# Three loads per pair of heads: one transfer of 128 rows each in place of two of 48, and the last pair taken second

## What is computed

```
f = 1 / (1 + exp(-f_logit))                      # batch 4, heads 8, seq 768, head_dim 48
for t in range(S):
    state = f[:, :, t, :, None] * state + einsum('bhd,bhe->bhde', k[:, :, t], v[:, :, t])
    y[:, :, t] = einsum('bhd,bhde->bhe', q[:, :, t], state)
x = y, heads side by side                        # (4, 768, 384)
x = first mixing network(x)                      # theta, cos/sin, token mixing, channel mixing
out = second mixing network(x)                   # w_in, normalise, w_spatial, gate, w_out
```

## Time and profile before

| | us |
|---|---|
| Median of 3 runs | 608.71 (608.22 to 608.74) |
| Profiled execution | 608.3 |
| Its span in the trace | 606.4 |
| Attention, until the mixing network runs alone | 0 to about 118 |
| Mixing networks | about 118 to 606.4 |

### The profile page before, as it was taken

How to read it: one execution, slowest core, us unless ns; L and a number is a source line. 1 busy time by engine, 2 the same in 40 slices (tenths; PEclk the granted TensorE clock), 3 DMA queues, 4 the chain that set the end, 5 groups by cost and what they waited for, 6 DMA issues and landing times.

```text
span 606.4 us, 11881 instructions
## 1 busy us (share of the span) xinstructions
PE 576.7 (95%) x4226; PEld 554.7 (91%) x4226; DVE 365.8 (60%) x614; ACT 289.9 (48%) x509; POOL 35.9 (6%) x66
## 2 busy tenths in 40 slices
PE   0898999999999999999999999999999999999997
PEld 0888888799988999999999999999999999989997
DVE  7899999677685456544855576557055704570240
ACT  5798999656453425333544345225221623253112
POOL 3233333100000000000000000000000000000000
PEclk9898999999999999999999999999999999999999
DMA  7889899486010221122013741200130011001102
GB/s 190 209 236 244 248 246 288 126 276 232 2 40 28 79 91 39 38 66 91 1 44 116 284 146 38 79 1 0 53 105 1 0 39 39 0 2 40 39 1 80
DMA packets 31113, 58.74 MB, mean 97 GB/s; under 512 B 3680, under 2 KB 23136, under 8 KB 30688
## 3 DMA queue, kind: packets, MB, share of 16 engines
q1 hardware_dynamic: 31072, 58.21, 31.5%
HBM read 44.04 MB, written 14.16 MB: 96 GB/s over the span
## 4 chain that ended last, share of the span: by engine, by line
PE 63%; DVE 5%; issue 3%; ACT 1%; DVEq 0%; ACTq 0%
PE gate_ps L1074 16%; PE ringc L1074 11%; PE small_ps L1074 10%; PE theta_bank L1074 9%; PE mix_ps L1537 5%; PE mix_ps L1542 5%; PE mix_ps L1538 5%; PE mix_ps L1074 1%; DVE stats L2069 1%; DVE w_lo L79 1%; PE small_ps L1501 1%; DVE z_lo L79 0%; DVE ang L1651 0%; DVE ang L1648 0%; DVE u L1693 0%
## 5 line engine op out<-in xcount | busy, mean ns | idle before, releaser
L1537 PE MATMUL mix_ps<-w_hi,z_hi 128*128 128x384 f32 x288 | 98.8, 343 | 0.7 <-DVE u L1693 0.7
L1538 PE MATMUL mix_ps<-w_lo,z_hi 128*128 128x384 f32 x288 | 96.7, 336 | 0.0
L1542 PE MATMUL mix_ps<-w_hi,z_lo 128*128 128x384 f32 x288 | 73.5, 337 | 0.0
L1074 PE MATMUL gate_ps<-w_hi 128*128 128x384 f32 x192 | 64.2, 334 | 0.0
L1074 PE MATMUL gate_ps<-w_hi,w_lo 128*128 128x384 f32 x192 | 64.2, 334 | 0.0
L1074 PE MATMUL gate_ps<-w_lo,w_hi 128*128 128x384 f32 x192 | 64.1, 334 | 0.0
L74 ACT ACTIVATE g_hi<-gate 128x384 fp32r<-128x384 f32 x32 | 16.9, 527 | 81.6 <-DVE gate L2119 81.6
L2115 DVE TENSOR_TENSOR gate<-gate_ps,b_all 128x384 f32<-128x384 f32 x32 | 17.8, 557 | 62.5 <-PE gate_ps L1074 62.5
L1537 PEld LDWEIGHTS mix_ps<-w_hi,z_hi 128*128 128x128 f32 x288 | 54.1, 188 | 1.2 <-DVE u L1693 1.1
L1538 PEld LDWEIGHTS mix_ps<-w_lo,z_hi 128*128 128x128 f32 x288 | 54.2, 188 | 0.0
L1542 PEld LDWEIGHTS mix_ps<-w_hi,z_lo 128*128 128x128 f32 x288 | 51.9, 188 | 0.2 <-DVE z_lo L79 0.2
(11 more groups left out here) (161 smaller groups left out, 1411.7 us busy)
## 6 DMA issues: line engine op xcount, KB each, us to landing
f_raw<-in_fT_dram SPq DMA_DIRECT2D x32, 144.0 KB, 3.6
k_raw<-in_kT_dram SPq DMA_DIRECT2D x32, 144.0 KB, 3.2
q_raw<-in_qT_dram SPq DMA_DIRECT2D x32, 144.0 KB, 3.7
v_raw<-in_vC_dram SPq DMA_DIRECT2D x16, 288.0 KB, 4.1
xT<-y_sb SPq DMA_DIRECT2D x32, 144.0 KB, 3.5
xt<-xT SPq DMA_DIRECT2D x8, 576.0 KB, 4.1
w_raw<-in_wB_dram SPq DMA_DIRECT2D x6, 768.0 KB, 6.1
u<-xT SPq DMA_DIRECT2D x8, 576.0 KB, 5.1
```

The costliest lines, as they stand in the source:

```text
L1074: done = pe.matmul(out, a, b, start=(first and n == 0), stop=(last and n == len(terms) - 1))
L1537: pe.matmul(out, z, w_hi[:, weights_of[r]], start=(s == 0 and r == 0), stop=False)
L1538: pe.matmul(out, z, w_lo[:, weights_of[r]], start=False, stop=False)
L1542: last = pe.matmul(out, part(z_lo[i], r * DMODEL + d * 128, 128), w_hi[:, weights_of[r]], start=False, stop=(s == ST - 1 and r == 1))
```

## The change

`f_raw`, `k_raw` and `q_raw` get 128 partitions (`LOADED`). One transfer fills all of them. Its source is a pattern written by hand over the DRAM tensor: 2 (a step of 48 rows), then 64 rows, then 768 values, so head 0 and the first 16 rows of head 1 go to partitions 0 to 63, and head 1 and the first 16 rows of the next pair to partitions 64 to 127. The destination is 128 partitions of 768 values. For the last pair these 16 rows would lie behind the end of the tensor, so it is loaded by two plain transfers, of 64 and of 48 rows. It is taken as step 1; step 0 stays pair 0, and steps 2 to 15 take pairs 1 to 14 (`taken`). Values and stores use the same order of pairs, their transfers are otherwise as before. The clearing of `f_raw`, `k_raw` and `q_raw` and the waits for it go. The load semaphores count 16 per load instead of 32, and one transfer more for buffer 1 (`rows_count`). The engines still work on partitions 0 to 111.

```diff
+LOADED = 2 * HEAD_AT[1]
-        f_raw = main.take("f_raw", [ROWS, SEQ], 2)
+        f_raw = main.take("f_raw", [LOADED, SEQ], 2)
...
-        f_in = [Count(nc, sems, f"f_in{i}", 32) for i in range(2)]
+        f_in = [Count(nc, sems, f"f_in{i}", 16) for i in range(2)]
...
+        def rows_count(c, p, i):
+
+            return half_count(c[i], p, 2) + 16 * i
...
-            def rows(raw, src, name, sem, p, b):
+            def taken(p):
+
                 if p.reg is None and p.const < 2:
-                    sp.wait_ge(cleared[name], b + 1)
-                for hd in range(2):
-                    sp.dma_start(raw[b % 2][HEAD_AT[hd]:HEAD_AT[hd] + HDIM, :],
-                                 src[p.times(1), hd * HDIM:(hd + 1) * HDIM, :]).then_inc(sem[b % 2].h, 16)
+                    return (0, PAIRS - 1)[p.const]
+                return p.times(1, -1)
+
+            def rows(raw, src, sem, p, b):
+                if p.reg is None and p.const == 1:
+
+                    for at, n in ((0, HEAD_AT[1]), (HEAD_AT[1], HDIM)):
+                        sp.dma_start(raw[b % 2][at:at + n, :], src[taken(p), at * HDIM // HEAD_AT[1]:at * HDIM // HEAD_AT[1] + n, :])\
+                          .then_inc(sem[b % 2].h, 16)
+                    return
+                heads_and_next = bass.AP(src.tensor, 0, [[PAIR * SEQ, PAIRS - 1], [HDIM * SEQ, 2], [SEQ, HEAD_AT[1]], [1, SEQ]])
+                sp.dma_start(raw[b % 2][:, :], heads_and_next[taken(p), :, :, :]).then_inc(sem[b % 2].h, 16)
...
-                             vC[p.times(1), :, :, :].rearrange("h p x -> p h x")).then_inc(v_in[b].h, 16)
+                             vC[taken(p), :, :, :].rearrange("h p x -> p h x")).then_inc(v_in[b].h, 16)
...
-            for i in range(2):
-                pool.memset(f_raw[i][:, :], 10.0).then_inc(cleared["f"], 1)
...
-            for i in range(2):
-                dve.memset(k_raw[i][:, :], 0.0).then_inc(cleared["k"], 1)
-                dve.memset(q_raw[i][:, :], 0.0).then_inc(cleared["q"], 1)
...
-                dve.wait_ge(q_in[i].h, half_count(q_in[i], p, 2))
-                if first(p):
-                    dve.wait_ge(cleared["q"], 2)
+                dve.wait_ge(q_in[i].h, rows_count(q_in, p, i))
```

More of the change, by code:

```diff
@@ L136, in ps @@
             return [ctx.enter_context(nc.psum_tensor(f"{name}{i}", [128, 512], F32)) for i in range(n)]
-        f_raw = main.take("f_raw", [ROWS, SEQ], 2)
+        f_raw = main.take("f_raw", [LOADED, SEQ], 2)
         cap = main.take("cap", [ROWS, SEQ], 2)
-        q_raw = main.take("q_raw", [ROWS, SEQ], 2)
-        k_raw = main.take("k_raw", [ROWS, SEQ], 2)
+        q_raw = main.take("q_raw", [LOADED, SEQ], 2)
+        k_raw = main.take("k_raw", [LOADED, SEQ], 2)
         csum = main.take("csum", [ROWS, SEQ], 2)
@@ L160, in attention @@
         cnt = lambda name, per, ahead=AHEAD: Count(nc, sems, name, per, ahead)
-        f_in = [Count(nc, sems, f"f_in{i}", 32) for i in range(2)]
-        q_in = [Count(nc, sems, f"q_in{i}", 32) for i in range(2)]
-        k_in = [Count(nc, sems, f"k_in{i}", 32) for i in range(2)]
+        f_in = [Count(nc, sems, f"f_in{i}", 16) for i in range(2)]
+        q_in = [Count(nc, sems, f"q_in{i}", 16) for i in range(2)]
+        k_in = [Count(nc, sems, f"k_in{i}", 16) for i in range(2)]
         v_in = [Count(nc, sems, f"v_in{i}", 16) for i in range(4)]
@@ L190, in attention @@
         y_sbd = cnt("y_sbd", 2)
-        cleared = {name: sems.enter_context(nc.semaphore(f"{name}_cleared")) for name in "fqk"}
         rest_cleared = sems.enter_context(nc.semaphore("rest_cleared"))
@@ L233, in _ @@
             m["open"]()
-            def rows(raw, src, name, sem, p, b):
+            def taken(p):
                 if p.reg is None and p.const < 2:
-                    sp.wait_ge(cleared[name], b + 1)
-                for hd in range(2):
-                    sp.dma_start(raw[b % 2][HEAD_AT[hd]:HEAD_AT[hd] + HDIM, :],
-                                 src[p.times(1), hd * HDIM:(hd + 1) * HDIM, :]).then_inc(sem[b % 2].h, 16)
+                    return (0, PAIRS - 1)[p.const]
[8 more added lines that the diff above has]
+                sp.dma_start(raw[b % 2][:, :], heads_and_next[taken(p), :, :, :]).then_inc(sem[b % 2].h, 16)
             def load_f(p, b):
                 sp.wait_ge(lg_done.h, lg_done.at(p.back(2), 1))
-                rows(f_raw, fT, "f", f_in, p, b)
+                rows(f_raw, fT, f_in, p, b)
             def load_rest(p, b):
                 sp.wait_ge(k_done.h, k_done.at(p.back(2), 1))
-                rows(k_raw, kT, "k", k_in, p, b)
+                rows(k_raw, kT, k_in, p, b)
                 sp.wait_ge(q_done.h, q_done.at(p.back(2), 1))
-                rows(q_raw, qT, "q", q_in, p, b)
+                rows(q_raw, qT, q_in, p, b)
                 sp.wait_ge(y_ps.h, y_ps.at(p.back(4), 2))
                 sp.dma_start(v[b][:, :].rearrange("p (h x) -> p h x", h=2),
-                             vC[p.times(1), :, :, :].rearrange("h p x -> p h x")).then_inc(v_in[b].h, 16)
+                             vC[taken(p), :, :, :].rearrange("h p x -> p h x")).then_inc(v_in[b].h, 16)
             def load_theta(p, b):
@@ L274, in store @@
                 for hd in range(2):
-                    sp.dma_start(xT[p.times(1), hd * HDIM:(hd + 1) * HDIM, :],
+                    sp.dma_start(xT[taken(p), hd * HDIM:(hd + 1) * HDIM, :],
                                  y_sb[i][HEAD_AT[hd]:HEAD_AT[hd] + HDIM, :]).then_inc(x_out[i].h, 16)
@@ L340, in neg_logs @@
                 act.wait_ge(top_done.h, top_done.at(p.back(2), 1))
-                act.activation(csum[i][:, :], f_raw[i][:, :], ACT.Exp, scale=-1.0).then_inc(lg_done.h, 1)
+                act.activation(csum[i][:, :], f_raw[i][0:ROWS, :], ACT.Exp, scale=-1.0).then_inc(lg_done.h, 1)
                 act.wait_ge(lg_done.h, lg_done.at(p, 1))
@@ L533, in keep_in_range @@
                 i = b % 2
-                dve.wait_ge(f_in[i].h, half_count(f_in[i], p, 2))
-                if first(p):
-                    dve.wait_ge(cleared["f"], 2)
-                dve.tensor_scalar(f_raw[i][:, :], f_raw[i][:, :], LOGIT_MIN, None, ALU.max).then_inc(f_kept.h, 1)
+                dve.wait_ge(f_in[i].h, rows_count(f_in, p, i))
+                dve.tensor_scalar(f_raw[i][0:ROWS, :], f_raw[i][0:ROWS, :], LOGIT_MIN, None, ALU.max).then_inc(f_kept.h, 1)
             def sums(p, b):
@@ L557, in scale_queries @@
                 i = b % 2
-                dve.wait_ge(q_in[i].h, half_count(q_in[i], p, 2))
-                if first(p):
-                    dve.wait_ge(cleared["q"], 2)
+                dve.wait_ge(q_in[i].h, rows_count(q_in, p, i))
                 dve.wait_ge(w_done.h, w_done.at(p, 1))
                 dve.wait_ge(y_ps.h, y_ps.at(p.back(4), 2))
-                dve.tensor_tensor(qs[b][:, :], q_raw[i][:, :], w_dn[i][:, :], ALU.mult).then_inc(q_done.h, 1)
+                dve.tensor_tensor(qs[b][:, :], q_raw[i][0:ROWS, :], w_dn[i][:, :], ALU.mult).then_inc(q_done.h, 1)
             def scale_keys(p, b):
                 i = b % 2
-                dve.wait_ge(k_in[i].h, half_count(k_in[i], p, 2))
-                if first(p):
-                    dve.wait_ge(cleared["k"], 2)
+                dve.wait_ge(k_in[i].h, rows_count(k_in, p, i))
                 dve.wait_ge(w_done.h, w_done.at(p, 2))
@@ L573, in scale_keys @@
                 dve.wait_ge(kt_ps.h, kt_ps.at(p.back(2), 1))
-                dve.tensor_tensor(ks[i][:, :], k_raw[i][:, :], w_up[i][:, :], ALU.mult).then_inc(k_done.h, 1)
+                dve.tensor_tensor(ks[i][:, :], k_raw[i][0:ROWS, :], w_up[i][:, :], ALU.mult).then_inc(k_done.h, 1)
             def scores_out(g):
```

## The result

| | us |
|---|---|
| Before, median of 5 runs | 608.71 (608.19 to 608.99) |
| After, median of 5 runs | 896.63 (896.04 to 897.35) |
| After, profiled execution and its span | 897.35, 895.5 |
| Ratio | 1.474, 95% interval 1.472 to 1.476 |

The account below looks back on a forecast made before the run. Before, the compute chain sets the attention's pace; after, two DMA engines: 361 + 39 + 2.6 + 1.5 us, sum 404, step 15's queries at about 408, a shift of 306; 608.3 + 306 = 914, median 915, range 850 to 1105.

Parts of the forecast that it names:

- The decisive step: Attention loads: each new transfer is cut at the source's outermost 2, so two engines carry 64 rows each, fourteen get nothing.
- Values and stores, 1.5 us each on an engine,: Attention's DMA queue: 18432 bytes per engine at 12.3 GB/s; 15 values and 11 stores before step 15's queries, 39 us.
- A load, 8.0 us,: Attention's DMA queue: 196608 bytes per engine at 24.5 GB/s; 45 full loads up to step 15's queries, 361 us.
- The end: From step 15's queries on: same work in the same order, so 0 us change, between -4 and +6.
- The queue that doesn't run dry: Attention: some 24 us of transfers stay queued, so the two engines never stand idle; period 27 us.
- All compute hides: Attention: a turn's 5.8 us of compute hides behind the 27 us period, at half of TensorE's clock too.
- The rivals with 16 engines: Attention loads: the cut follows the partitions, 16 shares of 8 rows; 607.2 or 616 us, chance 0.18 together.
- rival 2: Attention loads: all 16 engines, but 20% more bytes become the bound, 9 us more; 616 us, chance 0.10.
- rival 1: Attention loads: all 16 engines, transfers stay hidden, only the clears' gain remains; 607.2 us, chance 0.08.
- the missing clears: Kernel start: without the clears the first clipping can start earlier, gaining 0 to 2.1 us, taken as 1.5.
- Rival 3: Attention loads: two engines but slower, 16.1 GB/s, 12.2 us per load; 1103 us, upper part 0.1 of 0.82.
- Issues as worth nothing: SyncE in the attention: three loads save some 1.2 us of issuing per turn, but SyncE waits then, so no gain.

Follow-up runs that it names:

- the runs with 4, 7 and 8 groups: Changed kernel, each load's source cut into 4, 7 (on 112 partitions) or 8 groups in place of 2, other rows read: 723.5, 643.8 and 644.1 us.
- 16 groups: Changed kernel, each load's source cut into 16 groups of 8 rows in place of 2 of 64, other rows read: 615.35 us, ratio to before 1.012.
- the run with only the logits: Changed kernel, but only the logits come by the new one transfer; keys and queries by two plain transfers of 64 rows each: 722.6 us.

## Why the prediction was right

**The decisive step held:** each load of the changed kernel is cut in two and runs on two engines; its two reports and the share of 0.13 show it, and the runs with 4, 7 and 8 groups came within 5 us of what the same step gives for them (with 16 groups 5 to 8 us above it). The reason given for it, that only at the 2 can both sides be cut alike, was an argument, and which property of the two sides decides is shown for the source's count alone. The rule of the Trainium skill, "DMA: Bandwidth & Descriptors", section "Why a DMA increments its semaphore by 16 and not by 1", looks at both sides and gives two engines as well; in the source's count the runs agree with it, and the destination's was not varied by itself. Its rule to use one transfer of 128 partitions in place of two halves ("Rules for kernel authors") gains nothing here: with 16 engines on both sides, one issue took 615.35 us and two took 614.34.

**The size.** 915 was forecast, 897 measured, 18 less. The reports on the two engines give the terms one by one. One steady turn: logits at 199.40, keys at 207.43, queries at 215.23, values at 215.94, the store at 216.68, the next logits at 224.41. The queries of step 15 were forecast for 408 and are reported at 386.90, 21 less:

- *Values and stores, 1.5 us each on an engine,* is the term that was mis-sized. They take 0.7 each in this turn, 26 GB/s; the 26 in front of those queries take 20.3 us, not 39. The rate of 12.3 GB/s came from a stretch in which all 16 engines were at work, while here the other fourteen have passed their shares long before. This is 19 of the 21.
- *A load, 8.0 us,* was right. The three of this turn take 8.0, 7.8 and 7.7 us (25.2 GB/s at 7.8), and the mean of the 44 full loads behind the first is 7.95. All of them together are 3 us below the sum.
- The loads of step 1 take 3.1 us in place of 2.6, and the weights 1.75 in place of 1.5.

The last load is the slowest, 9.95 us. It runs from 376.95 on, when the other engines carry stores and the first pieces of the mixing network; in the run with only the logits a load was as slow with all sixteen at work. VectorE starts on it at once:

```profile
376.00:387.00 11.00, 0.79 (x16) 0.57 (x12) 0.08 (x1) 0.00 (x0) 0.00 (x0) 0.63 0.88 245
```
```profile
386.92 0.96 DVE L567 TENSOR_TENSOR qs<-q_raw,w_dn 112x768 f32<-112x768 f32 x1 [15.07 <-DMA q_raw<-in_qT_dram]
```

The rest of the way to 897 is 4 us more at the end, next, and 1 less because the median lies 0.7 us below the profiled execution, not 0.4 above.

**The end, taken as 0 with -4 to +6,** was +4. From these queries on 508.6 us are left (895.5 - 386.9), against 504.5. The mixing begins at

```profile
406.45 0.19 PEld L1539 LDWEIGHTS mix_ps<-w_hi,z_hi 128*128 128x128 f32 x1
```

19.5 us after the scaling, 16.4 before. In the stretch between, the granted clock is low at first:

```profile
380.00:393.00 13.00, 4.19 (x31) 3.69 (x33) 5.22 (x8) 2.54 (x5) 0.00 (x0) 0.50 0.74 216
```

0.50 is 1.2 GHz, after TensorE had stood idle for most of each turn; before, it ran at 1.00 in the same part (95 to 108 us). That the 3 us are this is likely; no run took it alone.

**The queue that doesn't run dry** held: in no microsecond from 4 to 386 is the share under 0.12; in the run with one slow load it held too. **All compute hides** held: the transposes, with the clock at 0.50 when a turn's work starts, take 404 ns on average in place of 278, and ScalarE waits at most 1.3 us for them.

**The rivals with 16 engines** can be judged by the run with two plain transfers: 614.3, and by the one with 16 groups, 615.4. The time of rival 2, bytes that are not hidden, fits better (616 forecast), and rival 1 would have been wrong by 7 us. Its sign was there to read, a DMA share of 1.00 in a full turn. It sized the bytes too high, 9 us where some 6 were lost, and both rivals gave the missing clears 1.5 us where, with rows loaded in their place, they bring 0; that was one of the two bounds named. Rival 3, slower engines, falls: each of the two moved 25.2 GB/s, not the 16.1 of a mixed stretch of all sixteen.

**Issues as worth nothing** was right as a gain. That they would become long was not foreseen.

## What to carry to other kernels

Before two transfers are merged into one, compare the outermost count of both sides. Sources that started with 2, 4, 7, 8 and 16 groups ran on 2, 4, 7, 8 and 16 engines here, so a pattern that starts with "2 halves" leaves fourteen idle. In a profile it is seen at once, as a flat DMA share (0.13 for 2 of 16) with all engines waiting. And where the DMA share of a turn is near 1.00, rows loaded only to fill a gap are not free (0.6 and 1.2% here); clears at the start that run beside the first loads gained nothing when 16 rows were loaded in their place.

## What was not expected of the hardware

- With slow transfers in the queue an issue held SyncE for 5 to 8 us (7.37 for one load above) where it takes 0.4 else; everything else that SyncE had to issue waited behind it. At 213.08, where the longest hold of this turn starts, six transfers are not yet fully reported: queries, values, two stores, logits and keys. Whether their number, their bytes or something else limits it is not shown.
- An engine's rate depends on what the others do. With two at work a full load takes 7.8 us, 25.2 GB/s; with all sixteen at work it took 9.9 (19.9 GB/s), in the last load of the changed kernel and in the run with only the logits. A short stretch of the kernel before had 24.5 with all sixteen at work, so being many is not enough to slow them; what is was not tested.
- The odd count 7 is used as it is: 643.8 us, against 644.1 with 8 and the same bytes per engine, and seven reports per load.
